# VectorE's round in the attention stage: order of the output scaling, the inverse sums and the low parts

## The chip, the cores and the metric

The kernel runs on one core of one Trainium2 chip. The metric is the device time of one execution in microseconds (us). Before the change it is 974.32 us, the median of three runs (973.99 to 974.92).

## The reference, cut to what matters

```python
scores = scale * q @ k.T                       # 32 heads (4 x 8), S = 576, D = 64
a = softmax(causal(scores)); local = a @ v
q_p = phi(q)                                   # phi(x) = x or exp(x)-1, plus 1
mem_out = (q_p @ M_prev) / (q_p @ z_prev + 1e-6)
attn = g * mem_out + (1 - g) * local           # g = sigmoid(beta), one per head
x = attn, heads side by side                   # 2304 tokens x 512
x = (silu(x @ w_gate) * (x @ w_val)) @ w_out   # d_ff 1536
out = act(x @ w_in) @ w_out2                   # d_ff 2048, act: 0 | (h+1)^2/4 | h
```

All in float32. The feed-forward products are formed from a high and a low part of each operand, three products for one, and with Strassen-like sums of quarters.

## The kernel before, in words

The program has two stages. The attention stage handles the 32 heads as NPAIR = 16 pairs; the feed-forward stage follows and fills the rest of the span. The five engines run programs of their own and meet by semaphores; on each engine (and in each DMA queue) the order is the order in which the program lists the instructions, and a wait holds up all that is listed behind it.

Each pair has four query tiles, 4 to 1 (tile i sees 64 + 128 i keys), and a short first block. A round p works on the scores of pair p and on the turning and the values of pair p-1. Step j = 4 p + 4 - i is tile i of pair p.

- TensorE in round p (L1533 to L1558): scores of tile 4 of pair p; the turns (transposes by a product with the identity) of pair p-1 in the order TURNS (L384): (4,0) (4,1) (3,0) (4,2) (3,1) (2,0) (1,0), then (2,1), the short block's scores, (1,1), the scores of tiles 3, 2, 1; then the values products of pair p-1. Turn groups go to PSUM banks 4 to 7 (BANK, L390): (3,0) to bank 7, then (4,2) to bank 6. The same two banks hold the values products of the pair before until VectorE has scaled them out (out_x, L1120): part 1 is bank 7, part 0 is bank 6. So the turn (3,0) waits for part 1 of the pair before and the turn (4,2) for part 0 (L1430 to L1433).
- ScalarE in round p: the copies of turned groups listed in ON_ACT (L385), the exponentials of pair p tile by tile (their row sums come out as rsum), then in some rounds one high part for the feed-forward stage (up_high, x_high), and at the start of the next round exp of q for the pair after.
- VectorE in round p (L1163 to L1197): sums_inverse (1 over the row sums of pair p-1), out_x of pair p-2 (parts 1 and 0), the copy of turned group (4,1), the row maxima of tile 4 (tile_max, which also moves the scores out of PSUM), the copy of (2,1), norm_q, the maxima of tile 3, rnorm_q, the maxima of tiles 2 and 1, the mem_scale of tiles 4, 3 and 2, phi of pair p+1; then in rounds 5, 6, 8 and 9 a low part of a weight piece (up_low, L1127) and in rounds 10 to 16 a low part of x (x_low, L1134); last the mem_scale of tile 1.
- GpSimd in its round p (L763 to L784): in rounds 2 to 7 sums of weight slots, in 8 and 9 a low part, in 10 to 13 a difference for x (x_sum, L755); then mem_rows of the four tiles, each behind its mem_scale (L694), phi_z of pair p+1, v_scale of pair p and relu_q of pair p+2.
- The inverse sums travel: they are turned by TensorE as a ninth-row group (L1441) behind the turn (1,0), copied to an SBUF row by ScalarE (rrow, L838), written to DRAM and read back spread over the partitions (rbc). out_x multiplies by rbc, so it waits for that read (L1123).
- SP issues the DMAs in one order (L605 to L613): for round p load_qk(p+1), load_nat(p+2), which waits until GpSimd has finished phi_z of pair p (L505), load_v(p), write_r(p-1), read_r(p-1). They share the queue q1.

The names that the change touches are ends_pair (L471), which says with which turn the inverse sums go, and the order inside VectorE's loop.

Of the kernel before, what the change touches and what calls it, by code (L numbers as in the profile page):

```python
# [14 lines left out]
def attention_two_ffns(nc, qk_in, nat_in, vm_in, beta, w_up, w_down, out):  # L15

    NPAIR = qk_in.shape[0]
# [33 lines left out]
    HIGH_AT = ((3, 0, 0), (4, 0, 1), (5, 0, 2), (6, 1, 0), (7, 1, 1), (8, 1, 2))  # L51
    X_SUMS_AT = ((10, 1), (11, 3), (12, 5), (13, 6))
    X_ORDER = (0, 2, 4, 1, 3, 5, 6)
    X_HIGH_AT = tuple((9 + n, X_ORDER[n]) for n in range(7))
# [5 lines left out]
    def width(i):  # L60

        return D + P * i

    def at_least(eng, sem, value):

        if value > 0:
            eng.wait_ge(sem, value)

    ctx = ExitStack()
    with ctx:  # L70
# [148 lines left out]
        def sums_before(u):  # L219

            return 4 * computed_before(u)
# [145 lines left out]
        def tile_of(j):  # L367

            return j // SLOTS, SLOTS - j % SLOTS

        def block_of(i, h):

            return 1 + 2 * (i - 1) + h
# [22 lines left out]
        def turned_count(j, g):  # L396

            p, i = tile_of(j)
            return len(TURNS) * p + TURNS.index((i, g)) + 1
# [13 lines left out]
        def values_count(j):  # L413

            p, i = tile_of(j)
            return SLOTS * p + VALUES.index(i) + 1

        def step_of(p, i):

            return SLOTS * p + SLOTS - i  # L420
# [47 lines left out]
        SCORE_F = 960  # L468


        def ends_pair(j, g):  # L471

            return tile_of(j)[1] == 1 and g == 0

        def r_rows(j):

            return ps[0:NBLK, group_bank(j, 0), 3 * P:4 * P]
# [326 lines left out]
        def _(act):  # L804
# [25 lines left out]
            def copy_pt(p, i, g):  # L830

                j = step_of(p, i)
                if j >= PTS:
                    act.wait_ge(pv_done, values_count(j - PTS))
                act.wait_ge(turned, turned_count(j, g))
                if ends_pair(j, g):
                    at_least(act, r_out, 32 * (p - 1))
                    nc.scalar.activation(rrow[0:NBLK, p % 2], r_rows(j), ACT.Copy).then_inc(r_row, 1)  # L838
                dst, src = group_ends(j, g)
                nc.scalar.activation(dst, src, ACT.Copy).then_inc(pt_act, 1)  # L840
# [38 lines left out]
            for p in range(NPAIR + 1):  # L879
                j = SLOTS * p  # L880
# [164 lines left out]
        def _(dve):  # L1045
# [23 lines left out]
            def tile_max(j):  # L1069

                p, i = tile_of(j)
                w = width(i)

                at_least(dve, scored, j + 2 if i == 2 else j + 1)
                for h in range(2):
                    t, k = 2 * j + h, block_of(i, h)
                    at_least(dve, expd, t - NEGS + 1)
                    col = score_col(i, h)
                    nc.vector.tensor_tensor_reduce(negs[:, t % NEGS, 0:w], psf[:, col:col + w],  # L1079
                                                   mask[:, S - w:S], -(float(D) ** -0.5), 3.0e38,  # L1080
                                                   ALU.add, ALU.min, nmax[:, p % 2, k:k + 1]).then_inc(maxed, 1)
                if i == 1:
                    at_least(dve, scoredf, p + 1)
                    at_least(dve, expdf, p - 1)
                    nc.vector.tensor_tensor_reduce(negf[:, p % 2], psf[:, SCORE_F:SCORE_F + D], maskf[:],
                                                   -(float(D) ** -0.5), 3.0e38, ALU.add, ALU.min,
                                                   nmax[:, p % 2, 0:1]).then_inc(maxedf, 1)

            def mem_scale(j):

                p, i = tile_of(j)
                at_least(dve, expd, 2 * (j + 1))
                if i == 1:
                    at_least(dve, expdf, p + 1)
                at_least(dve, q_rnorm, p + 1)
                at_least(dve, memd, j - SLOTS + 1)
                k = blocks_of(i)
                nc.vector.scalar_tensor_tensor(mscale[:, p % 2, k], rsum[:, p % 2, k], 1e-9, rnorm[:, p % 2, k],
                                               ALU.add, ALU.mult).then_inc(mscaled, 1)

            def sums_inverse(p):

                at_least(dve, expd, 2 * SLOTS * (p + 1))
                at_least(dve, expdf, p + 1)
                nc.vector.tensor_scalar(den[:, p % 2], rsum[:, p % 2], 1e-9, None, ALU.add).then_inc(dend, 1)
                at_least(dve, dend, p + 1)
                at_least(dve, turned, len(TURNS) * (p - 1))
                nc.vector.reciprocal(rden[:, p % 2], den[:, p % 2]).then_inc(rdend, 1)
# [11 lines left out]
            def out_x(p, part):  # L1120

                dve.wait_ge(pv_done, SLOTS * p + (2 if part == 1 else SLOTS))
                at_least(dve, r_in[p % 2], 32 * (p // 2 + 1))  # L1123
                dst, o, r = x_part(p, part)
                nc.vector.tensor_tensor(dst, o, r, ALU.mult).then_inc(x_done, 1)

            def up_low(u, n):  # L1127
                a, b = PIECES[n]
                dve.wait_ge(sums, sums_before(u) + (4, 3, 4)[n])
                dve.wait_ge(wu_hi[n], computed_before(u) + 1)  # L1130
                nc.vector.tensor_tensor(wu_l[u % 3][:, a:b], wu_r[u % 3][:, a:b], wu_h[u % 2][:, a - 1:b - 1].bitcast(F32),  # L1131
                                        ALU.subtract).then_inc(low_dve[n], 1)

            def x_low(sb, n):  # L1134

                dve.wait_ge(x_hi, x_count(sb, n))
                if sb == 0 and n in (1, 3):
                    dve.wait_ge(tp, 4 * sb + (2 if n == 1 else 4))
                src = {0: x_quarter(0, sb, 0), 2: x_quarter(1, sb, 0), 4: x_quarter(1, sb, 1)}
                nc.vector.tensor_tensor(xt_l[:, n], src[n] if n in src else raw_sum(sb, n),  # L1140
                                        xt_h[:, n].bitcast(F32), ALU.subtract).then_inc(x_lo, 1)
# [20 lines left out]
            tile_max(1)  # L1162
            for p in range(NPAIR + 2):  # L1163
                j = SLOTS * p
                if 0 < p <= NPAIR:
                    sums_inverse(p - 1)
                if p > 1:
                    out_x(p - 2, 1)
                    out_x(p - 2, 0)
                if 0 < p <= NPAIR:  # L1170
                    copy_pt(p - 1, 4, 1)
                if 0 < p < NPAIR:
                    tile_max(j)
                if 0 < p <= NPAIR:
                    copy_pt(p - 1, 2, 1)
                if p < NPAIR:
                    norm_q(p)
                    if p > 0:
                        tile_max(j + 1)
                    else:  # L1180
                        dve.wait_ge(gt_set, 3)
                    rnorm_q(p)
                    tile_max(j + 2)
                    mem_scale(j)
                    mem_scale(j + 1)
                    tile_max(j + 3)
                    mem_scale(j + 2)
                if p + 1 < NPAIR:
                    phi(p + 1)
                for m, u, n in HIGH_AT:  # L1190
                    if m == p - 1 and n > 0:
                        up_low(u, n)
                for m, n in X_HIGH_AT:
                    if m == p - 1:
                        x_low(0, n)
                if p < NPAIR:
                    mem_scale(j + 3)  # L1197

            def c11(u):
                at_least(dve, p1_c, u + 1)  # L1200
# [176 lines left out]
        def _(pe):  # L1377
# [43 lines left out]
            def turn(p, i, g):  # L1421

                j = step_of(p, i)
                at_least(pe, expd, 2 * (j + 1))
                at_least(pe, memd, j + 1)
                if i == 1:
                    at_least(pe, expdf, p + 1)
                if copied_under(j, g):
                    pe.wait_ge(*copied_under(j, g))
                if group_bank(j, g) == 7:  # L1430
                    at_least(pe, x_done, 2 * p - 1)
                if group_bank(j, g) == 6:
                    at_least(pe, x_done, 2 * p)  # L1433
                a, b = GROUPS[i][g]
                for c in range(a, b):
                    col = chunk_col(i, c)
                    mm = nc.tensor.transpose(ps[:, group_bank(j, g), (c - a) * P:(c - a + 1) * P],  # L1437
                                             rown[:, j % ROWN, col:col + P], ident[:])
                if ends_pair(j, g):
                    pe.wait_ge(rdend, p + 1)  # L1440
                    mm = nc.tensor.transpose(r_rows(j), rden[:, p % 2], ident[:])  # L1441
                mm.then_inc(turned, 1)
# [189 lines left out]
```

## Time and profile before

The profiled execution took 974.91 us, and its span, from the first to the last instruction, is 973.0 us.

| | busy us | share of the span |
|---|---|---|
| VectorE (DVE) | 692.2 | 71% |
| ScalarE (ACT) | 459.1 | 47% |
| GpSimd (POOL) | 336.2 | 35% |

The granted TensorE clock is 1.0 of full speed over the whole span. The attention stage takes the first 182 us or so; a round there is about 10.3 to 11 us. A timeline is read from the left: start, duration, engine, line, operation with output and inputs, count, and in brackets how long the engine was idle before it and what ended that. "SPq" is the issue of a DMA by SP, not its transfer.

### The profile page before, as it was taken

The page shows a single profiled execution, that of the slowest core. Times are in us where ns is not written, and L with a number is a line of the kernel's source. Part 1 is how long each engine was busy: PE and PEld are TensorE (multiplying, and loading weights), DVE is VectorE, ACT ScalarE, POOL GpSimd, SP SyncE. Part 2 cuts the span into 40 slices and gives each one's busy share as a digit, 9 for nine tenths or more (in the row PEclk, how much of TensorE's full clock was granted, in tenths as well). Part 3 has the DMA queues.
Part 4 walks back from the last instruction along what each step waited for, and adds up shares of the span by engine and source line. Part 5 has one row for each costly group of instructions (what it writes and reads, how often), then busy time and mean ns, then how long its engine had stood idle before and what let it go on. Part 6 is the DMA issues. An engine that isn't in the chain of part 4 may idle for free.

```text
span 973.0 us, 19123 instructions
## 1 busy us (share of the span) xinstructions
PE 963.2 (99%) x6372; PEld 927.0 (95%) x6372; DVE 692.2 (71%) x1369; ACT 459.1 (47%) x940; POOL 336.2 (35%) x385
## 2 busy tenths in 40 slices
PE   8999999999999999999999999999999999999998
PEld 7778777999999999999999999999999999999998
DVE  6788999476667555557555569888887677867766
ACT  7899888654444222234222246545543334433331
POOL 5777775287781000100000157798410010000000
PEclk9999999999999999999999999999999999999999
DMA  6554543698778655555555544767775754538421
GB/s 243 175 170 154 165 149 102 233 339 291 285 246 314 238 200 216 222 218 213 218 196 195 198 147 169 249 239 284 273 270 222 256 197 162 228 129 302 144 101 66
DMA packets 46158, 204.74 MB, mean 210 GB/s; under 512 B 5488, under 2 KB 5872, under 8 KB 46064
## 3 DMA queue, kind: packets, MB, share of 16 engines
q1 hardware_dynamic: 45920, 203.52, 57.5%
q8 instruction: 55, 0.90, 0.4%
q14 instruction: 39, 0.32, 0.1%
q10 hardware_dynamic: 144, 0.00, 0.0%
HBM read 147.33 MB, written 56.17 MB: 209 GB/s over the span
## 4 chain that ended last, share of the span: by engine, by line
PE 92%; DVE 3%; DMA 2%; issue 1%; ACT 1%; POOL 0%; SPq 0%; DVEq 0%; ACTq 0%; POOLq 0%
PE ps L1467 27%; PE ps L1469 26%; PE ps L1468 26%; PE ps L1437 5%; PE ps L1408 4%; PE ps L1461 4%; DVE negs L1079 1%; DMA wu_r<-w_up 1%; DMA qk<-qk_in 1%; PE ps L1418 0%; ACT rown L821 0%; DVE norms L1064 0%; DMA rbc<-rsums 0%; DVE xt_l L1140 0%; DMA rsums<-rrow 0%
## 5 line engine op out<-in xcount | busy, mean ns | idle before, releaser
L1467 PE MATMUL ps<-xt_h,wu_h 128*128 128x384 f32 x840 | 281.5, 335 | 0.7 <-DVE wu_l L1131 0.5
L1469 PE MATMUL ps<-xt_h,wu_l 128*128 128x384 f32 x840 | 280.7, 334 | 0.0
L1468 PE MATMUL ps<-xt_l,wu_h 128*128 128x384 f32 x840 | 280.7, 334 | 0.0
L1467 PE MATMUL ps<-hid_h,wd_h 128*128 128x384 f32 x672 | 225.0, 335 | 0.7 <-issue 0.6
L1469 PE MATMUL ps<-hid_h,wd_l 128*128 128x384 f32 x672 | 224.5, 334 | 0.0
L1468 PE MATMUL ps<-hid_l,wd_h 128*128 128x384 f32 x672 | 224.5, 334 | 0.0
L1258 DVE TENSOR_TENSOR xy<-xy,ps 128x384 f32<-128x384 f32 x288 | 158.2, 550 | 70.1 <-PE ps L1469 69.7
L935 ACT ACTIVATE hid_h<-hid_r 128x768 fp32r<-128x768 f32 x84 | 70.8, 843 | 205.0 <-DVE hid_r L1232 140.3
L1467 PEld LDWEIGHTS ps<-xt_h,wu_h 128*128 128x128 f32 x840 | 157.7, 188 | 2.8 <-issue 0.8
L1468 PEld LDWEIGHTS ps<-xt_l,wu_h 128*128 128x128 f32 x840 | 157.7, 188 | 0.0
L1469 PEld LDWEIGHTS ps<-xt_h,wu_l 128*128 128x128 f32 x840 | 157.7, 188 | 0.0
L1467 PEld LDWEIGHTS ps<-hid_h,wd_h 128*128 128x128 f32 x672 | 126.1, 188 | 2.1 <-issue 1.9
L1468 PEld LDWEIGHTS ps<-hid_l,wd_h 128*128 128x128 f32 x672 | 126.2, 188 | 0.0
L1469 PEld LDWEIGHTS ps<-hid_h,wd_l 128*128 128x128 f32 x672 | 126.1, 188 | 0.0
L1236 DVE TENSOR_TENSOR hid_l<-hid_r,hid_h 128x768 fp32r<-128x768 f32 x84 | 86.7, 1032 | 37.2 <-ACT hid_h L935 37.1
L755 POOL TENSOR_TENSOR traw<-xy 128x384 f32<-128x384 f32 x20 | 23.1, 1179 | 239.3 <-PE ps L1469 239.3
L821 ACT ACTIVATE rown<-negs,nmax 128x576 f32<-128x576 f32 (+3 forms) x128 | 77.0, 602 | 5.7 <-DVE nmax L1079 4.6
L920 ACT ACTIVATE u2s<-ps 128x384 f32<-128x384 f32 x60 | 29.4, 490 | 100.0 <-PE ps L1469 100.0
L720 POOL TENSOR_TENSOR wu_l<-wu_r,wu_h 128x256 fp32r<-128x256 f32 x65 | 55.1, 877 | 58.2 <-ACT wu_h L850 58.1
L1213 DVE TENSOR_TENSOR hb<-u2s,ps 128x384 f32<-128x384 f32 x60 | 33.1, 551 | 52.2 <-PE ps L1469 52.2
L1079 DVE CUSTOM_DVE_ANT_0 negs<-ps,mask 128x576 f32<-128x576 f32 (+3 forms) x128 | 65.8, 551 | 4.7 <-PE ps L1408 4.7
L1242 DVE SCALAR_TENSOR_TENSOR tmp<-tmp 128x768 f32<-128x768 f32 x48 | 52.0, 1083 | 23.8 <-ACT tmp L950 23.5
(87 smaller groups left out, 1291.3 us busy)
## 6 DMA issues: line engine op xcount, KB each, us to landing
wu_l<-kept_ul SPq DMA_DIRECT2D x40, 896.0 KB, 7.5
wu_h<-kept_uh SPq DMA_DIRECT2D x40, 896.0 KB, 5.5
kept_uh<-wu_h SPq DMA_DIRECT2D x20, 896.0 KB, 6.4
kept_ul<-wu_l SPq DMA_DIRECT2D x20, 896.0 KB, 7.5
wd_h<-kept_dh SPq DMA_DIRECT2D x28, 512.0 KB, 3.8
wd_l<-kept_dl SPq DMA_DIRECT2D x28, 512.0 KB, 5.5
wu_r<-w_up SPq DMA_DIRECT2D x20, 512.0 KB, 5.3
qk<-qk_in SPq DMA_DIRECT2D x15, 640.0 KB, 4.9
```

The source lines that it names most:

```text
L720: low = nc.gpsimd.tensor_tensor(wu_l[u % 3][:, k], wu_r[u % 3][:, k], wu_h[u % 2][:, k - 1].bitcast(F32), ALU.subtract)
L821: nc.scalar.activation(head_rows(j)[:, h + (i == 1), D:D + w], negs[:, t % NEGS, 0:w], ACT.Exp, bias=nmax[:, p % 2, k:k + 1], scale=-1.0, ...
L935: nc.scalar.activation(hid_h[:, t % 6], hid_r[:, t % 6], ACT.Copy).then_inc(hh_done, 1)
L1079: nc.vector.tensor_tensor_reduce(negs[:, t % NEGS, 0:w], psf[:, col:col + w], mask[:, S - w:S], -(float(D) ** -0.5), 3.0e38, ALU.add, ALU. ...
L1236: nc.vector.tensor_tensor(hid_l[:, t % 6], hid_r[:, t % 6], hid_h[:, t % 6].bitcast(F32), ALU.subtract).then_inc(hl_done, 1)
L1242: nc.vector.scalar_tensor_tensor(tmp[:, r], tmp[:, r], 1.0, tmp[:, r], ALU.min, ALU.mult).then_inc(s_done, 1)
L1258: nc.vector.tensor_tensor(y, y, o, ALU.add).then_inc(evac, 1)
L1408: mm = nc.tensor.matmul(psf[:, col + a0:col + a1], qk[rows, s, P + q0(i):P + q0(i) + P], qk[rows, s, P + S + a0:P + S + a1], start=True, s ...
L1437: mm = nc.tensor.transpose(ps[:, group_bank(j, g), (c - a) * P:(c - a + 1) * P], rown[:, j % ROWN, col:col + P], ident[:])
L1467: nc.tensor.matmul(dst, w_hi, v_hi, start=start, stop=False, skip_group_check=onto)
L1468: nc.tensor.matmul(dst, w_hi, v_lo, start=False, stop=False, skip_group_check=onto)
L1469: return nc.tensor.matmul(dst, w_lo, v_hi, start=False, stop=stop, skip_group_check=onto)
```

## The change

ends_pair is replaced by with_sums: the inverse sums are turned with group 0 of tile 2 (bank 5, one turn earlier) in place of group 0 of tile 1, and ScalarE copies the row before its copy of that group. In VectorE's round out_x part 1 comes first, then the mem_scale of tile 1 of the pair before (in the old order the last instruction of the round before), then sums_inverse, then out_x part 0. The low parts move from behind phi to between the maxima of tile 4 and the copy of (2,1).

```diff
-        def ends_pair(j, g):
-            return tile_of(j)[1] == 1 and g == 0
+        def with_sums(j, g):
+            return (tile_of(j)[1], g) == (2, 0)
...
-                if ends_pair(j, g):
+                if with_sums(j, g):
                     at_least(act, r_out, 32 * (p - 1))
                     nc.scalar.activation(rrow[0:NBLK, p % 2], r_rows(j), ACT.Copy).then_inc(r_row, 1)
...
             for p in range(NPAIR + 2):
                 j = SLOTS * p
+                if p > 1:
+                    out_x(p - 2, 1)
                 if 0 < p <= NPAIR:
+                    mem_scale(j - 1)
                     sums_inverse(p - 1)
                 if p > 1:
-                    out_x(p - 2, 1)
                     out_x(p - 2, 0)
                 if 0 < p <= NPAIR:
                     copy_pt(p - 1, 4, 1)
                 if 0 < p < NPAIR:
                     tile_max(j)
+                for m, u, n in HIGH_AT:
+                    if m == p - 1 and n > 0:
+                        up_low(u, n)
+                for m, n in X_HIGH_AT:
+                    if m == p - 1:
+                        x_low(0, n)
                 if 0 < p <= NPAIR:
                     copy_pt(p - 1, 2, 1)
...
                 if p + 1 < NPAIR:
                     phi(p + 1)
-                for m, u, n in HIGH_AT:
-                    if m == p - 1 and n > 0:
-                        up_low(u, n)
-                for m, n in X_HIGH_AT:
-                    if m == p - 1:
-                        x_low(0, n)
-                if p < NPAIR:
-                    mem_scale(j + 3)
...
-                if ends_pair(j, g):
+                if with_sums(j, g):
                     pe.wait_ge(rdend, p + 1)
                     mm = nc.tensor.transpose(r_rows(j), rden[:, p % 2], ident[:])
```

## Rows read from the trace of the kernel before

**Rows 1.** The page, busy us of each engine, its share and instructions.
```profile
PE 963.2 (99%) x6372; PEld 927.0 (95%) x6372; DVE 692.2 (71%) x1369; ACT 459.1 (47%) x940; POOL 336.2 (35%) x385
```

**Rows 2.** Waits of TensorE: us in total, times, longest.
```profile
PE ps L1437 <- DVE xy L1125: 2.0, 5, 0.5
```

**Rows 3.** Timeline of TensorE: starts of rounds 2, 11, 12, 15, 16, and turns.
```profile
24.68 1.30 PE L1408 MATMUL ps<-qk 64*128 64x512 f32 x8
...
118.17 1.30 PE L1408 MATMUL ps<-qk 64*128 64x512 f32 x8
...
129.12 1.30 PE L1408 MATMUL ps<-qk 64*128 64x512 f32 x8
...
131.90 2.09 PE L1437 MATMUL ps<-ident,rown 128*128 128x128 f32 x16 [0.45 <-DVE xy L1125]
133.82 0.27 PE L1441 MATMUL ps<-ident,rden 128*9 128x128 f32 x1
...
161.88 1.30 PE L1408 MATMUL ps<-qk 64*128 64x512 f32 x8
...
165.94 0.27 PE L1441 MATMUL ps<-ident,rden 128*9 128x128 f32 x1
...
172.21 1.09 PE L1437 MATMUL ps<-ident,rown 128*128 128x128 f32 x8
```

**Rows 4.** Timeline of VectorE, end of round 10 and first half of round 11.
```profile
118.88 1.16 DVE L1140 TENSOR_TENSOR xt_l<-xy,xt_h 128x768 fp32r<-128x768 f32 x1
119.96 0.15 DVE L1098 SCALAR_TENSOR_TENSOR mscale<-rsum,rnorm 128x3 f32<-128x3 f32 x1
...
120.36 0.77 DVE L1125 TENSOR_TENSOR xy<-ps,rbc 128x320 f32<-128x320 f32 x2
...
123.58 0.56 DVE L1117 COPY pt<-ps 128x384 f32<-128x384 f32 x1 [0.50 <-PE ps L1437]
...
126.06 1.01 DVE L1064 SCALAR_TENSOR_TENSOR norms<-norm,gt 128x9 f32<-128x9 f32 x1
```

**Rows 5.** Timeline of GpSimd, the tile 1 rows and the difference for x.
```profile
120.25 0.51 POOL L697 TENSOR_TENSOR rown<-qp,mscale 128x192 f32<-128x192 f32 x1 [1.03 <-DVE mscale L1098]
...
125.07 1.98 POOL L755 TENSOR_TENSOR xt_r<-xy,xt_r 128x384 f32<-128x384 f32 x2
```

**Rows 6.** Timeline of SP's DMA issues, nat and rbc of rounds 10, 11, 13.
```profile
111.34 0.34 SPq L506 DMA_DIRECT2D nat<-nat_in  x1
...
115.44 1.81 SPq L526 DMA_DIRECT2D rbc<-rsums  x2
...
122.31 0.34 SPq L506 DMA_DIRECT2D nat<-nat_in  x1
...
126.82 1.13 SPq L526 DMA_DIRECT2D rbc<-rsums  x2
...
144.19 0.34 SPq L506 DMA_DIRECT2D nat<-nat_in  x1
...
148.12 2.16 SPq L526 DMA_DIRECT2D rbc<-rsums  x2
```

**Rows 7.** Timeline of SP's rbc issue in round 7.
```profile
83.77 1.13 SPq L526 DMA_DIRECT2D rbc<-rsums  x2
```

**Rows 8.** Timeline of VectorE, out_x waiting for rbc, rounds 2 and 8.
```profile
26.54 0.82 DVE L1125 TENSOR_TENSOR xy<-ps,rbc 128x320 f32<-128x320 f32 x2 [0.87 <-DMA rbc<-rsums]
...
88.18 0.49 DVE L1125 TENSOR_TENSOR xy<-ps,rbc 128x320 f32<-128x320 f32 x1 [0.29 <-DMA rbc<-rsums]
```

**Rows 9.** The tile rbc: its 32 DMAs from issue to landing.
```profile
DMA to landing us min/median/max: 2.8/3.1/4.2
```

**Rows 10.** Timeline of ScalarE, the copy of the inverse sums in round 15.
```profile
166.34 0.25 ACT L838 ACTIVATE rrow<-ps 9x128 f32<-9x128 f32 x1
```

**Rows 11.** Timelines of GpSimd's relu_q and VectorE's norms in round 0.
```profile
11.27 1.65 POOL L669 TENSOR_SCALAR qrelu<-nat 128x576 f32<-128x576 f32 x1
...
12.20 0.17 DVE L1064 SCALAR_TENSOR_TENSOR norms<-norm,gt 128x9 f32<-128x9 f32 x1
```

## The prediction

> **What bounds the kernel now.** I began with the page: TensorE is busy for 99% of the span [rows 1], so whatever the change gives must come out of TensorE's waits or its round length. TensorE's waits, read next, have one line that the change touches: turns wait for out_x five times, 2.0 us in all [rows 2]. Its timeline shows where. A round counts from the scores of tile 4. From round 2 (24.68) to round 16 (172.21) are fourteen rounds in 147.53 us; an undisturbed one, round 15, takes 172.21 - 161.88 = 10.33, and 14 x 10.33 = 144.6, so 2.9 us are lost [rows 3]. Most of the loss lies in rounds 11 to 14: (161.88 - 118.17) / 4 = 10.93 each, 0.6 over [rows 3]. VectorE's timeline gives the reason there: behind phi stands a low part of x (1.16 us), then mem_scale, then the inverse sums, and out_x starts only at 120.36 [rows 4].
>
> Elsewhere the attention stage runs at TensorE's pace, with other chains close behind. I read one of these in full, through VectorE, GpSimd and SP, because the change puts new links into it.
>
> **The change part by part.**
>
> *Sums with tile 2.* The ninth-row turn is put before the three turns of (1,0), which take 0.12 us each (sixteen from 131.90 to 133.82 [rows 3]): the row is ready 0.36 earlier. In round 15 its copy starts at 166.34, 4.46 after the round's start [rows 3, 10]; it now starts at 4.10. The copy of (2,0) falls behind it, at most 0.25 late [rows 10]; bank 5 is needed again only behind the turns of (1,0) and (2,1), so I cost this at nothing, and at 0.25 a round at worst. The wait on rdend comes one turn earlier, with VectorE's inverse done more than 1 us before.
>
> *Low parts mid-round.* From behind phi to behind the maxima of tile 4: up to 1.16 us (the parts of x; those of weights are smaller) [rows 4] leave the stretch ahead of out_x and enter one where VectorE idled 0.50 us before the copy of (2,1) [rows 4]. Eleven rounds have one. What is not covered, 0 to 0.66 us, delays the maxima of tile 3 and the exponentials behind them, and reaches TensorE only where ScalarE has no idle time left. These rows don't price that: it is between 0 and 0.66 a round. I take 0, since ScalarE has idle time behind its copies in every round whose timeline I read, and keep 0.3 a round (3.3 us) for the range. Nor does it win anything beyond the 2.9 us above.
>
> *GpSimd beside it.* In round 11 norms took 1.01 us where it takes 0.17 elsewhere [rows 4, 11], and it ends at 127.07, just when GpSimd's two x_sum operations (125.07 to 127.05) end [rows 5]: a VectorE operation with two SBUF inputs waited for a GpSimd tensor_tensor. Mid-round, GpSimd is busy with v_scale and then relu_q. While relu_q ran (11.27 to 12.92), norms at 12.20 took its usual 0.17 [rows 11]: by that one row relu_q doesn't hold VectorE up. The Trainium skill ("SBUF — State Buffer", Who interferes with whom) says otherwise: a VectorE instruction with two SBUF inputs contends with any GpSimd instruction that reads SBUF, and whichever came second is blocked until the first has finished. By that rule each low part could wait for up to 1.65 us of relu_q; by the row it waits for v_scale's tail only. I go by the row; the rule is the third rival.
>
> *out_x part 1 ahead of mem_scale.* This is the step that decides. Before, mem_scale of tile 1 waited for exponentials only. Now it stands behind out_x part 1, which waits for rbc. And GpSimd's rows of tile 1 wait for mem_scale, phi_z is queued behind these rows, SP's load_nat waits for phi_z, and behind load_nat in SP's order and in the one queue stand load_v, the writing of the sums and the reading of rbc for the next pair, for which the next round's out_x part 1 waits. The chain closes: one turn of it is one round. Its length L from out_x start to out_x start:
> - out_x part 1 after a wait 0.41 (0.82 for two [rows 8]), then mem_scale to GpSimd's start 0.29 (119.96 to 120.25 [rows 4, 5]): 0.70.
> - GpSimd's start to the issue of nat: 122.31 - 120.25 = 2.06 [rows 5, 6].
> - nat's issue to rbc's first issue. In the four rounds 10 to 13 the sums' row is ready soon after nat, as it will be now, and the gap is 4.10, 4.51, 3.98 (round 12, not shown) and 3.93 [rows 6]: the sums' packets stand behind those of nat and vm. Mean 4.13; I take 4.1.
> - rbc's first issue to the waiting out_x: 88.18 - 83.77 = 4.41 [rows 7, 8]. The second issue starts 0.6 later, and a landing takes 2.8 to 4.2 [rows 9], so it is 3.4 to 4.8; I take 4.1, the middle.
>
> L = 0.70 + 2.06 + 4.1 + 4.1 = 10.96, against TensorE's 10.33. With all four at their least (3.93 and 3.4) it is 10.1, with the greatest 12.1; the mean of many rounds is narrower, 10.6 to 11.3.
>
> What slack does it meet? TensorE reaches the turn into bank 7 at 2.13 of its round (the sums' turn is at 165.94 - 161.88 = 4.06, and 133.82 - 131.90 = 1.92 after that point), bank 6 four turns later, at 2.61 [rows 3]. From out_x part 1 to the end of part 0 are 0.41 + 0.40 (mem_scale and the inverse, 119.96 to 120.36 [rows 4]) + 0.41 = 1.22, and about 0.12 to TensorE's start. So TensorE stalls when out_x part 1 starts later than 1.27 of the round. In round 2 it starts at 26.54 [rows 8], which is 1.86: the slack is gone at once, since that round's rbc is behind the weight loads. From there the chain leads. With O the start of out_x part 1, the next round starts at O + 10.33 - 1.27 = O + 9.06. Twelve turns, up to the last round with a nat load ahead of it: O(14) = 26.54 + 12 x 10.96 = 158.1, round 15 starts at 167.1 against 161.88 [rows 3]: 5.2 us later. From there no nat is loaded, rbc comes early enough, and rounds 15 and 16 keep their lengths. The 2.9 us of stalls are contained in this; they lie in the new wait's shadow.
>
> *The end of the stage.* The last rbc gates the last out_x and VectorE's part in the first feed-forward step, not TensorE; against TensorE it comes 0.36 earlier. Nothing lost, nothing won; if it did hold TensorE it would be some tenths. The feed-forward stage is the same code, bound by TensorE.
>
> **Sum.** 974.91 + 5.2 = 980.1 for a profiled execution; this one is 0.59 above the median, so 974.32 + 5.2 = 979.5.
>
> **The rivals.**
>
> First, the other side: the chain stays under 10.33. It needs both DMA links near their least (3.93 + 3.6 gives 10.29). Then out_x part 1 is early, the low part is out of its way, and TensorE's losses go but for some 0.5 us: 974.3 - 2.4 = 971.9. For it speaks that all of these lengths vary, and that the sums' row comes 0.36 earlier, which is inside the chain only if the row is the later of the two. Against it: no single round shows both links that short, and it needs the mean of twelve. It decides from L = 10.5 downwards: each 0.1 in L is 1.2 us, and at 10.53 the change is even.
>
> Second, a weak chain: L of 10.5 to 10.6, because the write of the sums, issued closer behind nat, gets in with less delay. 26.54 + 12 x 10.55 + 9.06 = 162.2: 974.6, no change.
>
> Third, the lock by relu_q as in the rule above: each low part in nine rounds (5, 6, 8, 9 and 10 to 14) would come up to 1.1 us later. What reaches TensorE I estimate from rounds 11 to 14, where VectorE's chain was 0.84 longer (norms, 1.01 against 0.17) and the round 0.6: some 5 us in nine rounds. Without the chain that gives 974.3 - 2.4 + 5 = 976.9; with it most lies in the chain's shadow, and the time is 979.5 to 982.
>
> **How the numbers follow.** A difference of 0.2%, 1.9 us, is about what can be told from no change. The forecast (the chain leads, with or without a little from the low parts) has 0.68, the lock as the larger part 0.06, the weak chain 0.11, the gain 0.15. The forecast's own range is 976.5 (L = 10.7) to 983 (L = 11.2 with 0.1 us a round of uncovered low parts). Leaving 0.13 below and 0.07 above, the range is 973.5 to 983.5. Slower by over 0.2% (above 976.3): 0.74; within: 0.12; faster: 0.14.
>
> **What would show it.** Right: rounds 3 to 14 of 10.7 to 11.2 us, TensorE's turns waiting for out_x (L1125's new line) in nearly all of them, VectorE's longest wait being out_x for rbc, and from nat's issue to the rbc issue about 4.1, with the nat issue about 4.6 into the round. The x_sum blocking of norms may go or stay without effect. Wrong in the main step: rounds of 10.33 with out_x waiting little, nat at 3 to 3.5 into the round. Wrong in the lock: low parts of over 2 us that end with relu_q. Wrong in the turn of the sums: TensorE waiting for ScalarE's copy of (2,0).

## The result, and the profile after

The changed kernel takes 980.81 us (median of 5 runs, 980.42 to 983.38) against 974.8 us for the kernel before on the same chip (973.99 to 974.94, 5 runs). The ratio over all runs is 1.0068, 95% interval 1.0057 to 1.0079 (the two medians alone give 1.0062): slower by 6 us. The prediction was 979.5, 5.2 us slower, with a range of 973.5 to 983.5.

The profiled execution of the kernel after took 981.66 us, 6.75 more than the one of before, at a granted clock of 1.0 in both. The page, busy us of each engine, answers to [rows 1]: TensorE is "busy" for 2.7 us more though it does the same work (its ends are modelled), GpSimd for 4.3 more.

```profile
PE 965.9 (99%) x6372; PEld 927.2 (95%) x6372; DVE 693.0 (71%) x1369; ACT 460.8 (47%) x940; POOL 340.5 (35%) x385
```

Waits of TensorE and of VectorE after (us in total, times, longest). They answer to [rows 2, 8]. The first line has grown from 2.0 us in five waits to 4.4 in eight. VectorE's wait for rbc is the large one: 15 of its 16 pairs have it, 23.7 us in total against 5.7 in three before. 5.2 and 4.6 of it are the last pair's wait, behind which no further round follows.

```profile
PE ps L1437 <- DVE xy L1125: 4.4, 8, 0.9
PE ps L1408 <- DVE nmax L1085: 2.3, 5, 1.4
...
PE ps L1437 <- ACT pt L840: 0.3, 1, 0.3
```

```profile
DVE xy L1125 <- DMA rbc<-rsums: 23.7, 15, 5.2
```

The same line before:

```profile
DVE xy L1125 <- DMA rbc<-rsums: 5.7, 3, 4.6
```

TensorE's timeline after, starts of rounds 5, 6, 7, 11, 14, 15 and 16, with one turn that waits; it answers to [rows 3].

```profile
56.74 1.30 PE L1408 MATMUL ps<-qk 64*128 64x512 f32 x8
...
67.79 1.30 PE L1408 MATMUL ps<-qk 64*128 64x512 f32 x8
...
71.06 1.86 PE L1437 MATMUL ps<-ident,rown 128*128 128x128 f32 x13 [0.95 <-DVE xy L1125]
...
79.54 0.70 PE L1408 MATMUL ps<-qk 64*128 64x512 f32 x2
...
124.56 1.30 PE L1408 MATMUL ps<-qk 64*128 64x512 f32 x8 [0.24 <-DVE nmax L1085]
...
157.96 1.30 PE L1408 MATMUL ps<-qk 64*128 64x512 f32 x8 [0.20 <-DVE nmax L1085]
...
168.46 1.30 PE L1408 MATMUL ps<-qk 64*128 64x512 f32 x8
...
178.80 1.09 PE L1437 MATMUL ps<-ident,rown 128*128 128x128 f32 x8
```

Round 5 takes 11.05 us, round 6 11.75. Rounds 4 to 13, from 45.44 to 157.96, take 11.25 each; rounds 14 and 15 are back at 10.50 and 10.34. From round 2 (24.65) to round 16 are 154.15 us against 147.53: 6.6 of the 6.75 us. The line of waits alone would have shown 2.4 of them. Most of the rest is in TensorE's modelled busy time (2.7), in waits for nmax (0.9) and for a ScalarE copy (0.3); a round's length counts it all.

One turn of the chain, round 10 to 11. VectorE's timeline, then GpSimd's, then SP's; they answer to [rows 4 to 6].

```profile
115.23 0.49 DVE L1125 TENSOR_TENSOR xy<-ps,rbc 128x320 f32<-128x320 f32 x1 [1.57 <-DMA rbc<-rsums]
115.64 0.15 DVE L1098 SCALAR_TENSOR_TENSOR mscale<-rsum,rnorm 128x3 f32<-128x3 f32 x1
115.71 0.17 DVE L1105 TENSOR_SCALAR den<-rsum 128x9 f32<-128x9 f32 x1
...
118.28 1.72 DVE L1140 TENSOR_TENSOR xt_l<-xy,xt_h 128x768 fp32r<-128x768 f32 x1
...
126.07 0.49 DVE L1125 TENSOR_TENSOR xy<-ps,rbc 128x320 f32<-128x320 f32 x1 [0.72 <-DMA rbc<-rsums]
```

```profile
115.93 0.51 POOL L697 TENSOR_TENSOR rown<-qp,mscale 128x192 f32<-128x192 f32 x1 [2.02 <-DVE mscale L1098]
...
116.68 1.29 POOL L679 TENSOR_TENSOR qz<-qp,nat 128x512 f32<-128x512 f32 x1
117.91 1.27 POOL L687 TENSOR_TENSOR vm<-vm,cf 128x640 f32<-128x640 f32 x1
119.14 2.36 POOL L669 TENSOR_SCALAR qrelu<-nat 128x576 f32<-128x576 f32 x1
```

```profile
117.99 0.34 SPq L506 DMA_DIRECT2D nat<-nat_in  x1
118.37 0.43 SPq L511 DMA_DIRECT2D vm<-vm_in  x1
118.84 0.69 SPq L517 DMA_DIRECT2D rsums<-rrow  x1
...
121.86 1.53 SPq L526 DMA_DIRECT2D rbc<-rsums  x2
```

ScalarE's timeline, the copy of the sums' row in the same round:

```profile
117.99 0.25 ACT L838 ACTIVATE rrow<-ps 9x128 f32<-9x128 f32 x1
```

Read across VectorE, GpSimd and SP: out_x waits for rbc and starts at 115.23; 0.70 later GpSimd has mem_scale and starts; 2.06 later SP may issue nat; 3.87 later the sums are in DRAM and rbc is issued; 4.21 later the next out_x starts. It took 10.84 here and 11.18 in the mean of the twelve turns.

A second way leads from out_x to the same write, which the prediction did not follow: the turns into banks 7 and 6 wait for out_x, and behind them TensorE turns the sums and ScalarE copies the row. That copy starts at 117.99, in the same moment as nat's issue; the write goes out only behind nat and vm. If nat and vm weren't ahead of it, I estimate from e6 (write 0.28 behind the start of the row's copy, rbc's issue 2.35 later) a turn by this way of 2.76 + 0.28 + 2.35 + 4.25 = 9.64 us, less than TensorE's 10.33. e1 and e6 leave this way whole, and the loss is gone in both.

### The profile page after: what moved, and what is told of

It reads as the page before. It is cut to its first block, busy times and chain, and to the rows that moved or that the text cites. A ratio compares the mean times of both kernels' runs of the same rounds, so it can differ in the third digit from the quotient of the medians.

```text
span 979.8 us, 19123 instructions
## 1 busy us (share of the span) xinstructions
PE 965.9 (99%) x6372; PEld 927.2 (95%) x6372; DVE 693.0 (71%) x1369; ACT 460.8 (47%) x940; POOL 340.5 (35%) x385
## 4 chain that ended last, share of the span: by engine, by line
PE 85%; DMA 5%; DVE 3%; issue 3%; POOL 2%; SPq 1%; ACT 1%; DVEq 0%; ACTq 0%; POOLq 0%
PE ps L1467 26%; PE ps L1469 25%; PE ps L1468 25%; DMA rbc<-rsums 3%; PE ps L1437 3%; PE ps L1408 2%; PE ps L1461 2%; DMA rsums<-rrow 2%; DVE negs L1079 1%; POOL qz L679 1%; DMA wu_r<-w_up 1%; DVE xt_l L1140 1%; SPq L517 0%; PE ps L1384 0%; ACT xt_h L871 0%
## 5 line engine op out<-in xcount | busy, mean ns | idle before, releaser
L1242 DVE SCALAR_TENSOR_TENSOR tmp<-tmp 128x768 f32<-128x768 f32 x48 | 52.0, 1083 | 23.7 <-ACT tmp L950 23.5
L1437 PE MATMUL ps<-ident,rown 128*128 128x128 f32 x464 | 63.3, 277 | 5.3 <-DVE xy L1125 4.4
```

The source lines that it names most:

```text
L1242: nc.vector.scalar_tensor_tensor(tmp[:, r], tmp[:, r], 1.0, tmp[:, r], ALU.min, ALU.mult).then_inc(s_done, 1)
```

## The experiments

Twelve experiments were run (e10 is the kernel of e1 a second time), each beside the kernel before on the same chip. The kernel before had medians of 975.1 (first four), 975.0 (next four), 974.78 (e9 to e11) and 974.98 (e12). The groups ran on different chips, so a difference between experiments of two groups, or to the kernel after, is uncertain by some tenths.

### e1: mem_scale ahead of out_x part 1

From the kernel after; the rest of the change stays.

```diff
+                if 0 < p <= NPAIR:
+                    mem_scale(j - 1)
                 if p > 1:
                     out_x(p - 2, 1)
                 if 0 < p <= NPAIR:
-                    mem_scale(j - 1)
                     sums_inverse(p - 1)
```

> The changed kernel with one swap: mem_scale of tile 1 stands ahead of out_x part 1 again; the sums with tile 2 and the low parts mid-round stay. Theory (closed chain rbc, out_x, mem_scale, phi_z, nat load, rbc): the link from rbc to GpSimd is cut, rounds 2 to 15 go back to 10.3 to 10.5 us, nat is issued 3 us into the round, and the time is 972 to 974. Rival (the low parts mid-round, blocked by and blocking GpSimd, make the loss): nothing of that is removed, the time stays at 979 to 981. Rival (the sums' row with tile 2 costs): also 979 to 981.

Measured: 975.46 us (11 runs, 973.61 to 976.4), ratio 1.0001 (0.9993 to 1.001). 5.4 of the 6 us are gone by taking one 0.15 us instruction from behind the wait for rbc. The median lies 1.5 over the 972 to 974 that I expected, and the runs spread over 2.8 us; e9, e10 and e12 are about that. The profiled execution is the fastest of the eleven, and its twelfth round is long all the same (11.47 us). VectorE's timeline of e1 there:

```profile
131.16 0.49 DVE L1125 TENSOR_TENSOR xy<-ps,rbc 128x320 f32<-128x320 f32 x1 [1.66 <-DMA rbc<-rsums]
131.57 0.16 DVE L1105 TENSOR_SCALAR den<-rsum 128x9 f32<-128x9 f32 x1
```

rbc lands late, and out_x starts 2.54 into the round.

### e2: nat loaded last

From the kernel after, SP's order alone: the loop stays open because rbc is issued before nat.

```diff
-                if p + 2 < NPAIR:
-                    load_nat(p + 2)
...
                     read_r(p - 1)
+                if p + 2 < NPAIR:
+                    load_nat(p + 2)
```

> The changed kernel, VectorE's order untouched; SP issues load_nat behind the write and the read of the sums in place of ahead of them. Theory: the chain is cut at its other link, rbc no longer stands behind nat, out_x waits little, rounds of 10.3 to 10.5 us, time 972 to 974, although mem_scale still stands behind out_x. Rival (out_x first is late because of the sums' own way through DRAM, whatever nat does): rbc comes no earlier than before, time 978 to 981. Rival (low parts): 979 to 981.

Measured: 979.42 us (5 runs, 977.73 to 982.17), ratio 1.0044 (1.003 to 1.0058). The link itself did change. SP's timeline of e2, round 4:

```profile
51.12 0.69 SPq L517 DMA_DIRECT2D rsums<-rrow  x1
...
53.48 1.13 SPq L526 DMA_DIRECT2D rbc<-rsums  x2
54.65 0.58 SPq L506 DMA_DIRECT2D nat<-nat_in  x1
```

From the write's issue to rbc's are 2.36 us where the kernel after has 3.02 (118.84 to 121.86), and TensorE's waits for out_x fell to one of 0.4 us. But nat is now 3.5 us behind the write, and ScalarE's exp of q, which heads its next round, waits for it, with the copies of turned groups behind. ScalarE's timeline and TensorE's longest line of waits in e2:

```profile
58.54 0.69 ACT L810 ACTIVATE qexp<-nat 128x576 f32<-128x576 f32 x1 [0.56 <-DMA nat<-nat_in]
```

```profile
PE ps L1437 <- ACT pt L840: 4.7, 7, 1.7
```

The theory's time (972 to 974) is missed. 979.42 lies where both rivals had it, but the first rival's reason, rbc no earlier than before, is not what the trace shows, and the second, the low parts, is left to e4. I had taken away one wait and made another. So e2 decides nothing about the chain, and e6 asks the question again.

### e3: only the order in front of out_x

From the kernel before: out_x part 1, then mem_scale of tile 1, then the inverse, then part 0. The low parts stay behind phi, the sums with tile 1.

```diff
+                if p > 1:
+                    out_x(p - 2, 1)
                 if 0 < p <= NPAIR:
+                    mem_scale(j - 1)
                     sums_inverse(p - 1)
                 if p > 1:
-                    out_x(p - 2, 1)
                     out_x(p - 2, 0)
...
-                if p < NPAIR:
-                    mem_scale(j + 3)
```

> The kernel before with out_x part 1 ahead of mem_scale and the inverse sums, and nothing else of the change: sums with tile 1, low parts behind phi. Theory: this part alone carries the loss; rounds of about 11.2 us from 3 to 14, time 980 to 983 (the sums come 0.4 us later than in the changed kernel, and the low parts stand ahead of out_x, but both are in the shadow of the wait for rbc). Rival (low parts or sums): about 975.

Measured: 980.65 us (5 runs, 979.48 to 981.66), ratio 1.006 (1.0046 to 1.0074). This part alone gives the whole loss: the whole change, at 980.81, can't be told from it. The part moves mem_scale and the inverse sums together; e1 and e9 take them apart.

### e4: only the low parts mid-round

From the kernel before: the two loops over HIGH_AT and X_HIGH_AT moved to behind tile_max(j), nothing else.

> The kernel before with the low parts moved mid-round and nothing else. Theory: 972.5 to 974.5: the stalls of rounds 11 to 14 (2.9 us with the others) go in part, and no chain is closed. Here relu_q will be in progress when VectorE asks for the low part. If relu_q holds VectorE up, low parts take over 2 us and end 0.6 to 0.9 us behind relu_q's start plus 1.65; the time is then 975 to 979. If it doesn't, low parts take 0.66 to 0.95 us. Rival (low parts make the loss): 979 to 981.

Measured: 972.61 us (9 runs, 972.36 to 973.33), ratio 0.9976 (0.9967 to 0.9986): 2.5 us faster, and the fastest kernel of the study beside e7 and e8, which contain it. TensorE's waits for out_x are down to 1.2 us in two. Two low parts and the GpSimd operations beside them, VectorE's and GpSimd's timelines of e4:

```profile
60.12 0.80 DVE L1131 TENSOR_TENSOR wu_l<-wu_r,wu_h 128x512 fp32r<-128x512 f32 x1
...
111.89 1.46 DVE L1140 TENSOR_TENSOR xt_l<-xy,xt_h 128x768 fp32r<-128x768 f32 x1
```

```profile
59.70 1.65 POOL L669 TENSOR_SCALAR qrelu<-nat 128x576 f32<-128x576 f32 x1
...
111.88 1.64 POOL L669 TENSOR_SCALAR qrelu<-nat 128x576 f32<-128x576 f32 x1
```

Unheld, the first shape takes 0.69 us and the second 0.95 (e11 has both, below and at 71.27). So the first, 0.42 after relu_q's start, lost 0.11, and the second, 0.01 after it, lost 0.51: both could go on some 0.5 us after relu_q had begun, more than 1 us before its end. One that comes 0.83 after relu_q's start (133.87 and 133.04) takes its usual 0.95.

### e5: only the sums with tile 2

```diff
-            return tile_of(j)[1] == 1 and g == 0
+            return (tile_of(j)[1], g) == (2, 0)
```

> The kernel before with the inverse sums turned with tile 2 and nothing else. Theory: cost and gain near nothing, 974.5 to 975.5 (the row comes 0.36 us earlier, VectorE's part is unchanged and still makes rounds 11 to 14 0.6 us long). Rival (this edit carries the 2.9 us by which the swapped kernel, mem_scale first, lies above the one with low parts mid-round alone): 976.5 to 978.

Measured: 975.26 us (11 runs, 974.48 to 976.54), ratio 1.0002 (0.9994 to 1.0011). Nothing; its one trace is a wait of 0.3 us for a ScalarE copy.

### e6: a third buffer for nat

From the kernel after, with both orders untouched. load_nat(p) then waits for the phi_z of one pair earlier, long done, so nat is no longer a link of the loop.

```diff
-        nat, a = place("nat", [P, 2, NBLK + 3, D], F32, a)
+        nat, a = place("nat", [P, 3, NBLK + 3, D], F32, a)
...
-                at_least(sp, q_z, 2 * (p - 1))
+                at_least(sp, q_z, 2 * (p - 2))
...
```

nat's semaphores and every use of its buffers go from two to three in the same way.

> The changed kernel with a third buffer for nat, so that load_nat of pair p+2 waits for phi_z of pair p-1 and not of pair p. VectorE's order and SP's order are untouched; the chain from mem_scale to the nat load is gone, and no load comes late, as it did when nat stood behind the read of the sums. Theory: rbc issue 2.3 to 2.5 us behind the write of the sums, rounds of 10.3 to 10.5, time 972.5 to 976. Rival (mem_scale behind out_x costs by itself, by GpSimd's late start): 978 to 981.

Measured: 973.76 us (11 runs, 972.84 to 974.55), ratio 0.9983 (0.9975 to 0.9992): 7 us less than the kernel after. SP's timeline of e6, and VectorE's:

```profile
64.22 0.43 SPq L506 DMA_DIRECT2D nat<-nat_in  x1
...
70.55 0.69 SPq L517 DMA_DIRECT2D rsums<-rrow  x1
...
72.90 1.13 SPq L526 DMA_DIRECT2D rbc<-rsums  x2
```

```profile
67.27 0.49 DVE L1125 TENSOR_TENSOR xy<-ps,rbc 128x320 f32<-128x320 f32 x1 [0.65 <-DMA rbc<-rsums]
```

nat goes 6.3 us ahead of the sums, and the write takes 2.35 to rbc's issue. out_x still waits for rbc, but 1.08 into its round (66.19), inside the slack of 1.27. The loop is cut at a quite different link than in e1, and the loss goes both times; e7 shows that the third buffer wins nothing where the loop is open already. That the loop is the cause is shown.

Not all rounds are at 10.3 to 10.5, as I had expected: the eleventh takes 11.59 and the twelfth 10.79, with out_x 2.26 and 1.47 into them. e1 (twelfth, 11.47) and e4 (eleventh and twelfth, 11.18 and 10.85) have it there too: rbc lands late in these rounds with the loop open as well. Why was not tested.

### e7 and e8: on top of the low parts

e7 is e4 with e6's third buffer, e8 is e4 with e5's line.

> The low parts mid-round alone plus the third nat buffer. Theory: the nat load leaves the way of the sums, rbc lands earlier and the remaining waits of TensorE for out_x (1.2 us in two rounds) go: 971 to 972.6. Rival (those waits came from VectorE's own queue): 972.6 as without the third buffer.

> The low parts mid-round plus the sums with tile 2; out_x stays behind mem_scale and sums_inverse. It separates what the swapped kernel (975.5) had over the low parts alone (972.6). If the sums with tile 2 carry it: 975 to 976. If the inverse sums standing behind out_x part 1, and so behind rbc, carry it: 972.3 to 973.

Measured: e7 972.74 us (7 runs, 972.56 to 973.09), ratio 0.9974 (0.9964 to 0.9985); e8 972.99 us (9 runs, 972.3 to 973.5), ratio 0.9976 (0.9966 to 0.9986). Neither can be told from e4. The buffer is worth something only where the loop leads, the turn of the sums nowhere.

### e9: the inverse sums behind out_x part 1

e1 and e8 differ in one thing left, where the inverse sums stand. e9 is e4 with that alone.

```diff
+                if p > 1:
+                    out_x(p - 2, 1)
                 if 0 < p <= NPAIR:
                     sums_inverse(p - 1)
                 if p > 1:
-                    out_x(p - 2, 1)
                     out_x(p - 2, 0)
```

> The low parts mid-round alone, plus the inverse sums behind out_x part 1 (mem_scale stays at the end of the round, the sums stay with tile 1). The swapped kernel took 975.5 where the low parts with the sums of tile 2 took 973.0; what lies between them is that the inverse sums stand behind out_x part 1. If the inverse sums' place carries it: 974 to 976, with TensorE waiting in single rounds where rbc lands late. If not (it is mem_scale's place at the start of the next round): 972.3 to 973.

Measured: 975.43 us (11 runs, 973.95 to 978.03), ratio 1.0009 (1.0 to 1.0018), 2.8 over e4 by the medians (each against its own kernel before, 3.1), and with 4.1 us more widely spread than e1. Two rounds of its profile are long, the seventh with 11.31 us and the fourteenth with 11.52. VectorE's timeline in them, and GpSimd's:

```profile
78.31 0.49 DVE L1125 TENSOR_TENSOR xy<-ps,rbc 128x320 f32<-128x320 f32 x1 [0.83 <-DMA rbc<-rsums]
78.71 0.95 DVE L1105 TENSOR_SCALAR den<-rsum 128x9 f32<-128x9 f32 x1
...
79.83 0.38 DVE L1125 TENSOR_TENSOR xy<-ps,rbc 128x256 f32<-128x256 f32 x1
...
152.59 1.17 DVE L1105 TENSOR_SCALAR den<-rsum 128x9 f32<-128x9 f32 x1
```

```profile
78.36 1.27 POOL L679 TENSOR_TENSOR qz<-qp,nat 128x512 f32<-128x512 f32 x1
...
152.46 1.27 POOL L679 TENSOR_TENSOR qz<-qp,nat 128x512 f32<-128x512 f32 x1
```

den, 0.17 us long in the kernel before, ends both times within 0.04 us of GpSimd's phi_z (79.66 and 79.63; 153.76 and 153.73). So it is held by it, and out_x part 0 stands behind it. In the kernels before and after all 16 den take 0.16 to 0.18 us: before, den is done ahead of out_x, before phi_z starts; after, mem_scale stands directly ahead of den and GpSimd starts only when den has (115.71 and 115.93). The changed order thus avoids this block, and pays with the loop. e6, which has that order and no loop, bears this out: every den takes 0.17 us there, and its 973.76 is 0.8 over e8.

The Trainium skill ("SBUF — State Buffer", Who interferes with whom) lists tensor_scalar among the VectorE operations that can take the port pair shared with GpSimd, if their operands meet certain conditions, and says that the second to come blocks until the first has finished. Here the trace agrees: 0.95 and 1.17 us, ending with phi_z.

### e10: e1 once more

> The swapped kernel (mem_scale first) once more for its profile: its first profiled execution (973.6) was the fastest of eleven, whose median is 975.5. Theory: in a slower execution two or three rounds are 0.5 to 1 us longer, each after an rbc that landed 0.5 us or more later than in the first profile. Rival: the difference lies outside the attention stage.

One execution: 975.27 us against 974.78, and 1.66 over the first profile of e1. At the start of round 15 it is 1.57 behind that one (162.37 against 160.80), so nearly all of the difference lies in the attention stage. 0.47 of it is a wait for qk (0.8 us) ahead of round 2, 0.84 is round 2 (11.17 against 10.33), 0.27 is round 12 (11.74 against 11.47).

In round 2 out_x starts 1.70 into the round where the first profile has 1.07, so rbc was 0.6 later, and den took 0.70 where it took 0.16: as I had expected, with the block of e9 on top. In round 12 rbc was not later (2.36 against 2.54), but den took 0.60 where it took 0.16. So a late rbc makes a long round by itself, as e1's twelfth shows, and den's block behind it makes it longer. Two profiles are few: how much of the 2.8 us of spread either of them carries is not shown.

### e11: relu_q ahead of v_scale

From e4: GpSimd does relu_q first, then v_scale.

> The low parts mid-round alone, with GpSimd's relu_q ahead of v_scale, so that VectorE asks for its low part in the first third of v_scale (a tensor_tensor, 1.26 us) and not in relu_q. If a GpSimd tensor_tensor holds the second SBUF input from start to end: parts of x take 1.7 to 2.1 us and end 0.95 us behind v_scale's end. If it is held only at the start, as relu_q seems to (low parts asked 0.4 to 0.6 us into it took 0.80 and 0.96 us): 0.95 to 1.3 us. The time should be 973 to 975 in the first case, 972 to 973 in the second.

One execution: 973.78 us against 974.78. It was meant to tell which GpSimd operation holds VectorE and until when. VectorE's timeline of e11, and GpSimd's:

```profile
60.75 1.78 DVE L1131 TENSOR_TENSOR wu_l<-wu_r,wu_h 128x512 fp32r<-128x512 f32 x1
...
112.89 0.95 DVE L1140 TENSOR_TENSOR xt_l<-xy,xt_h 128x768 fp32r<-128x768 f32 x1
```

```profile
60.73 1.26 POOL L687 TENSOR_TENSOR vm<-vm,cf 128x640 f32<-128x640 f32 x1
...
111.41 1.66 POOL L669 TENSOR_SCALAR qrelu<-nat 128x576 f32<-128x576 f32 x1
113.03 1.94 POOL L687 TENSOR_TENSOR vm<-vm,cf 128x640 f32<-128x640 f32 x1
```

A low part 0.02 us behind v_scale's start takes 1.78 where 0.69 is usual, so it waited nearly to v_scale's end. One 1.48 us into relu_q takes its usual 0.95, and then v_scale, asked for while the low part runs, takes 1.94 where 1.26 is usual. Only two low parts met v_scale's start, fewer than I had set it up for.

### e12: the inverse sums behind both parts

From e9: sums_inverse stands behind out_x part 0, ahead of the copy of (4,1).

```diff
                 if p > 1:
                     out_x(p - 2, 1)
-                if 0 < p <= NPAIR:
-                    sums_inverse(p - 1)
-                if p > 1:
                     out_x(p - 2, 0)
+                if 0 < p <= NPAIR:
+                    sums_inverse(p - 1)
```

> As the version with the inverse sums behind out_x part 1 (975.43), but they now stand behind both parts of out_x. In that version's profile the two long rounds (7 and 14, 11.31 and 11.52 us) each have the first operation of the inverse sums (den, 128x9, 0.17 us alone) take 0.95 and 1.17 us, ending with GpSimd's phi_z, with out_x part 0 behind it. Theory, the operand port: that blocked operation ahead of part 0 is what the order costs. Behind part 0 it may still be blocked by up to 1.2 us, but delays only the copy of (4,1), which has some 0.75 us of idle time ahead of it: 972.6 to 973.6, narrow again, turns waiting for out_x 1.2 us or less in all, and den still up to 1.2 us long in rounds where rbc comes late. Rival, the late rbc itself costs (the inverse sums are a further 0.4 us on a path that rbc leads, the port is no part of it): the sums' turn is then as late as before, and the time stays at 974.8 to 976 with the same wide spread.

Measured: 976.08 us (10 runs, 974.93 to 976.75), ratio 1.0009 (1.0 to 1.0019). den was held as the port theory says (0.98 us here, up to 1.21), but the time is the rival's, and a little over it. VectorE's timeline of e12, GpSimd's, and TensorE's, tenth round:

```profile
111.28 0.82 DVE L1125 TENSOR_TENSOR xy<-ps,rbc 128x320 f32<-128x320 f32 x2 [0.48 <-DMA rbc<-rsums]
112.02 0.98 DVE L1105 TENSOR_SCALAR den<-rsum 128x9 f32<-128x9 f32 x1
...
113.17 0.64 DVE L1117 COPY pt<-ps 128x512 f32<-128x512 f32 x1
```

```profile
111.69 1.28 POOL L679 TENSOR_TENSOR qz<-qp,nat 128x512 f32<-128x512 f32 x1
```

```profile
113.95 0.84 PE L1438 MATMUL ps<-ident,rown 128*128 128x128 f32 x6 [0.71 <-DVE pt L1117]
```

My step that the copy of (4,1) had 0.75 us to spare was wrong: a turn waits for it. That wait is new (2.5 us in six, 0.7 the longest), and this round took 11.21 us. The rounds of more than 10.5 us are 2, 3, 6, 7, 10 and 12; in the first five den took 0.56 to 1.19, in the twelfth 0.33 behind an out_x that waited 1.12 for rbc, and in all the others den took 0.28 or less. So the block is real and goes with the long rounds here; but rbc is late in the same rounds, and what each of the two costs isn't split by these runs. The spread, 1.8 us, is narrower than in e1 and e9, which the rival had not foreseen.

## Why the prediction was right, and where its terms were off

**The bound and the step that decides** held. The predicted loop is in the trace link by link, e3 shows that this part of the change alone makes the loss, and e1 and e6 cut the loop at two different places and both get it back.

**The length of the loop** was forecast as 10.96 and is 11.18, from the start of out_x at 24.89 to that at 159.07 over 12. By link: out_x and mem_scale to GpSimd 0.70 and on to nat 2.06, together 2.75 in the mean, against 2.76; nat to rbc 4.18 against 4.1 (3.86 to 4.75); rbc's issue to out_x 4.25 against 4.1 (3.56 to 4.69). The last had been taken as the middle between two ends; it lies above it. Over twelve turns the 0.22 make 2.7 us.

**Where the loop starts** was off the other way. I took out_x of round 2 at 26.54 as given [rows 8]. After, it is at 24.89, 1.65 less, because rbc was issued at 21.15 in place of 22.47. The order ahead of out_x is not the reason: before, VectorE had stood idle for 0.87 waiting for that rbc. How much of it the change makes isn't shown, since this landing varies by itself: e1 and e10 are one kernel, and out_x of round 2 is at 25.73 in one and at 26.83 in the other.

**Together**: the prediction's start of round 15, 167.1, less 1.65, plus 2.7, plus 0.3 gives 168.46 as measured. The 0.3 is that the last out_x of the loop (159.07) came 1.11 into round 14, before the slack of 1.27 was used up, so that the round's length counts from its own start, and that this round took 10.50 and not 10.33. The predicted 5.2 us became 6.6 in the profile and 6.0 between the medians. The two errors partly cancelled: a right start with the loop as I had it would have given 3.6, a right loop with the start as I had it 7.9. The path, the sign and the size of some us were foreseen; that the number came within 1 us is partly luck. e3, with the sums still at tile 1, shows the sum with both terms as I had them: out_x of round 2 at 26.48, a turn of 10.94 in the mean, round 15 at 166.80.

**The range of round lengths**, 10.7 to 11.2 for rounds 3 to 14, was missed at both edges: round 3 took 10.45, rounds 4 to 13 10.76 to 11.80 with a mean of 11.25, round 14 10.50. nat's issue lies 4.2 to 5.4 into its round, forecast 4.6. "Turns waiting for out_x in nearly all of them" is too strong: TensorE shows eight such waits, in seven of the twelve rounds.

**The low parts mid-round** were costed at nothing and contained in the 2.9 us of stalls. e4 shows what that is: alone they win 2.5, and they win nothing where the loop leads (e3 against the kernel after). That the stalls "lie in the new wait's shadow" held, by the same comparison.

**The sums with tile 2** at nothing: right (e5, e8).

**The inverse sums** behind out_x were in my sum only as 0.40 us between the two parts. With the low parts mid-round and mem_scale in its old place that order costs 2.8 (e9). In the kernel after it is not paid as such, since den escapes the block there; e6, with the same order, is 0.8 over e8.

**The lock, the third rival.** Low parts did grow, up to 1.72 where 0.95 is usual, but not to over 2 us and not to relu_q's end. At 118.28 above, x_low waits for v_scale (117.91 to 119.18) and then holds relu_q, which was queued behind v_scale and takes 2.36 where 1.65 is usual. What I read from one row, that relu_q doesn't hold VectorE up, is right only from 0.5 us after its start on (e4). That a low part waits "for v_scale's tail only" was right. By the rule of the Trainium skill (same page and section) relu_q would hold a low part that comes second for its whole 1.65 us; the trace doesn't agree, 1.46 at 111.89 in e4, which is 0.51 over the unheld 0.95.

## What to carry to other kernels

Before an instruction is put behind one that waits for a transfer, follow what the moved one releases, engine by engine and through the DMA queue, and see whether the path returns to that same transfer: if it closes, its length is a lower bound of the round, however idle each engine in it is. Where a 0.15 us instruction stood cost 5.4 of the 6 us here. And price each part alone: this change held one part worth 2.5 us, which showed only when the others were taken away.

## What the runs showed of the hardware

- A GpSimd tensor_tensor holds VectorE's low parts, and den, nearly from its own start to its end: a low part took 1.78 where 0.69 is usual (60.75 in e11), and den up to 1.21 where it is 0.17 (e12).
- GpSimd's relu_q, a tensor_scalar of 1.65 us, holds a low part for its first 0.5 us only. Low parts that came 0.01, 0.22 and 0.42 us after its start (111.89, 101.57 and 60.12 in e4) took 1.46, 0.99 and 0.80 where 0.95, 0.69 and 0.69 are usual: each was free 0.52 to 0.53 after that start.
- VectorE's two-input operations are not the only ones held: den has one input of 9 elements a partition, and waited up to 1.04 us (e12).
- Between two queued GpSimd operations a waiting VectorE one gets in first, and the second GpSimd one then waits for all of it: relu_q took 2.36 us where 1.65 is usual (after), v_scale 1.94 where 1.26 is (e11).
- The write of the sums, 9 x 128 floats in two DMAs, took 2.35 us from its first issue to the issue that waits for it in nearly all rounds of e6, where no load stands just ahead of it, and 3.0 to 3.9 in the kernel after, issued 0.8 to 1.4 us behind nat.
